# Attention and two MLPs on one core: own buffers for the first batch's queries and keys, the first weight split on three engines, unread products on TensorE

## The chip, the cores and the metric

The kernel runs on one core of a Trainium2 chip. The metric is the device time of one execution in microseconds. The engines are TensorE (PE in the profile, its weight loads PEld), VectorE (DVE), ScalarE (ACT), GpSimd (POOL) and SyncE (SP), which here issues all transfers. Each runs its own list of instructions in order and waits on semaphores.

## The reference

Causal attention with a bias of cumulated sums, over 4 batches of 8 heads, 576 tokens and a head dimension of 64, then two MLPs over the 2304 tokens (512 wide).

```python
scores = scale * np.matmul(q, k.transpose(0, 1, 3, 2))      # q, k, v: (4, 8, 576, 64)
cum = np.cumsum(np.maximum(s, 0.0), axis=-1)
bias = -(cum[:, :, :, None] - cum[:, :, None, :])
scores = np.where(causal, -1000000000.0, scores + np.minimum(bias, 0.0))
x = softmax(scores) @ v                                      # then to (2304, 512)
...
h = x @ w_in                                                 # first MLP, 1024 wide
solu = h * softmax(h)
ln = (solu - mean(solu)) / np.sqrt(var(solu) + 1e-06) * g_ln
x = ln @ w_out
...
h = x @ w2_in                                                # second MLP, 2048 wide
out = (h * np.clip(h + 3.0, 0.0, 6.0) / 6.0) @ w2_out
```

## The kernel before, in words

Products of float32 values are made of three products of rounded parts: each operand is split in a part "hi" (rounded to the type fp32r that TensorE takes) and a part "lo" (the rest), and hi·hi, hi·lo and lo·hi are added up in PSUM. So each weight and each activation has a split: a copy or cast that rounds, and a subtraction.

**Attention in slots.** The work goes by units. A unit is a pair of heads of one batch and one of two kinds: the first kind takes the first 256 queries (two slots), the other the remaining 320 (five slots). There are 32 units, eight for each batch (four of the first kind, then four of the other), and 112 slots. `BASE[u]` is the first slot of unit `u`. Every engine runs a loop over the slot number `n`, and its order in a slot is written out by hand. In slot n TensorE transposes the probabilities of slot n (`transpose_probs`, L687), spreads the reciprocals (`scales`, L724), multiplies with the values (`weighted_values`, L712), does a part of the first MLP, and computes the scores of slot n + 2 (`scores`, L668, L671 for the mask, L673). ACT copies slot n's transposes (L1088) and takes the exponentials of slot n + 1 (L1065). DVE takes the row maximum of slot n + 1 with the bias added (L884) and subtracts for the low part of the probabilities (L893).

**Queries and keys.** They come by `load_qk` on SP, one load for each unit and head of the pair (`load_of(u, e)` = 2u + e), into three buffers in turn, with a wait until the scores of the load three before are done. ACT rounds them (`split_qk`, L1057), POOL subtracts for queries (L555) and keys (L558). `SPLIT_AT` names the slot.

**The bias.** DVE sums s up (L864, L866), SP stores the sums to memory (L473), and loads them back spread over 128 partitions (`load_bias`, L446), behind a wait for the store.

**The first MLP.** It goes in 18 tiles of 128 tokens, from slot 14 on: tile t starts at slot `STARTS[t]` and takes six steps, spread over the slots up to the next start. Steps 0 to 2 are the hidden products (`hidden`, L742: 24 products of 512 columns), steps 3 to 5 the softmax and, from the third tile on, the products with w_out for an earlier tile (`project`, L771). Its input's split is on DVE (L939) and POOL (`split_x`, L604). The weight w_in (512 x 1024) is loaded in four transfers in slots 0, 2, 4, 6. POOL splits it alone, in 16 parts of 256 columns (`split_w_in`: cast L589, subtraction L591), one or two in each slot from slot 3 on; the first hidden product waits for all 16. w_out (L932 on DVE, L1101 on ACT) is split in slots 24 to 31.

**The second MLP** follows behind slot 134 and has TensorE nearly to itself.

Of the kernel before, what the change touches and what calls it, by code (L numbers as in the profile page):

```python
# [14 lines left out]
P = 128  # L15
# [4 lines left out]
F1 = 1024  # L20
# [63 lines left out]
STARTS = [14, 23] + [32 + 7 * i for i in range(4)] + [60 + 6 * i for i in range(8)] + [109, 116, 122, 128, 134]  # L84
# [7 lines left out]
W_IN_PARTS = 16  # L92
W_IN_FROM, W_OUT_FROM, EARLY_FROM = 3, 24, 120

# [40 lines left out]

SUMS_AT = {}
# [34 lines left out]
def build(nc, qk0, qk1, v_rows, s, w_in, w_out, g_ln, w2_in, w2_out, cum_dram, out):  # L171
    with ExitStack() as ctx:
# [35 lines left out]
        qk_hi, qk_raw, qk_lo = [], [], []  # L208
        for p in range(3):
            qk_hi.append(sb(a_region, f"qk_hi{p}", [P, ST], F32R))  # L210
            with nc.sbuf_tensor(f"qk_raw{p}", [P, ST], F32) as raw:
                qk_raw.append(raw)
            qk_lo.append(sb(a_region, f"qk_lo{p}", [P, ST], F32R))
# [16 lines left out]
        w_in_lo = sb(first, "w_in_lo", [P, NC, F1], F32R)  # L230
        w_out_hi = sb(first, "w_out_hi", [P, NF1, DM], F32R)
# [106 lines left out]
        qk_loaded = [sem(f"qk_loaded{p}") for p in range(3)]  # L338
# [4 lines left out]
        w_in_loaded = [sem(f"w_in_loaded{p}") for p in range(NC)]  # L343
# [31 lines left out]
        w_in_split = sem("w_in_split")  # L375
# [43 lines left out]

        def tokens(u):  # L420

            b, p, c = u // (2 * PAIRS), u % PAIRS, kind(u)
            return p, slice(SEQ * b + Q0[c], SEQ * b + Q1[c])

        @block.sync
        def _(sp):
            def load_qk(u, e):
                load = load_of(u, e)
                p, c = load % 3, kind(u)
                if load >= 3:  # L430
# [37 lines left out]

            sp.dma_start(s_pos[:, :], s).then_inc(s_loaded, 16)
# [12 lines left out]
            first_tail = min(u for u in range(UNITS) if not FIRST_KIND[u])  # L482
            load_bias_tail(first_tail)
            for n in range(-2, BASE[UNITS] + 4):

                for load in range(3, 2 * UNITS):
# [47 lines left out]
        def _(pool):  # L534
# [12 lines left out]
            def split_qk(u, e, behind):  # L547

                load, c = load_of(u, e), kind(u)
                p = load % 3  # L550
# [33 lines left out]
            def split_w_in(n):  # L584
                width = NC * F1 // W_IN_PARTS
                raw, hi, lo = (t[:, :, :].rearrange("p c f -> p (c f)")[:, n * width:(n + 1) * width]
                               for t in (w_in_raw, w_in_hi, w_in_lo))
                pool.wait_ge(w_in_loaded[n * NC // W_IN_PARTS], 16)
                pool.tensor_copy(hi, raw).then_inc(w_in_hi_done, 1)  # L589
                pool.wait_ge(w_in_hi_done, n + 1)  # L590
                pool.tensor_tensor(lo, raw, hi.bitcast(F32), ALU.subtract).then_inc(w_in_split, 1)  # L591
                return w_in_split, n + 1
# [24 lines left out]
            w_in_next = 0  # L617
            for n in range(-3, END + 1):
                t, r = STEP_AT.get(n, (None, None))
                if n in SPLIT_X_AT:  # L620
                    behind = split_x(SPLIT_X_AT[n])
# [3 lines left out]
                for u, e in VALUES_AT.get(n, ()):  # L625
                    behind = split_v(u, e)
                if r == 5:
# [17 lines left out]
        def _(pe):  # L645
            def scores(n, part=None):
# [12 lines left out]
                for tile, e, _ in TILES[n]:  # L659
# [3 lines left out]
                    p = load_of(u, part if e is None else e) % 3  # L663
# [148 lines left out]

            pe.wait_ge(consts_done, 4)
            pe.wait_ge(mask_tail_done, 2)
            pe.wait_ge(zeros_done, 1)
            for n in range(-2, END):
# [14 lines left out]
                if 0 <= n + 2 < ITEMS:  # L831
# [5 lines left out]
                    if k == 2:  # L837
                        scores(n + 4, 0)
                if r in (1, 2):
# [22 lines left out]
        def _(dve):  # L862
# [7 lines left out]
            def row_max(n, tile, e, col):  # L870
# [5 lines left out]
                else:  # L876
                    dve.wait_ge(bias_loaded[e][half_of(u)], 16 * len(units_of_half(u)))
# [37 lines left out]
            def scale_pair(u):  # L915
# [12 lines left out]
                last.then_inc(x_done, 1)  # L928

# [52 lines left out]
            for n in range(-2, END + 1):  # L982
# [25 lines left out]
                if n in X_AT:  # L1008
                    split_x(X_AT[n])
# [224 lines left out]
```

## Time and profile before

| | |
|---|---|
| median of 3 runs | 928.36 us (926.16 to 928.52) |
| the profiled execution | 927.4 us, span 925.6 us |
| TensorE busy | 846.5 us (91%), 4912 matmuls |
| DVE, ACT, POOL busy | 437.2, 407.7, 307.9 us |
| granted TensorE clock, mean | 0.972 of 2.4 GHz |

The span is what the profiler saw of the program on the core; the time of the execution has 1.8 us more around it. Busy times are of one execution. A line such as L742 is the line of the kernel that the instruction comes from. The row of a group ends with the idle time of the engine in front of it and what ended it.

### The profile page before, as it was taken

What the parts mean: (1) busy time and instruction counts of PE and PEld (TensorE: products, weight loads), DVE (VectorE), ACT (ScalarE), POOL (GpSimd) and SP (SyncE); (2) the same over time, 40 slices, a digit from 0 to 9 for tenths busy, and PEclk for the clock granted to TensorE, in tenths of its full rate; (3) what the DMA queues carried; (4) which work ended last, traced back from release to release, by engine and by line L of the source; (5) the groups of instructions that cost most, each with busy time, mean ns of one, the idle gap of its engine ahead of it and who ended that gap; (6) DMA issues with size and microseconds to landing.
All of it is one profiled execution on the core that took longest, in us unless ns stands there. A gap on an engine that the chain in (4) does not pass through costs nothing.

```text
span 925.6 us, 13793 instructions
## 1 busy us (share of the span) xinstructions
PE 846.5 (91%) x4912; PEld 753.1 (81%) x4912; DVE 437.2 (47%) x1057; ACT 407.7 (44%) x901; POOL 307.9 (33%) x419
## 2 busy tenths in 40 slices
PE   5676878999899998999898999999999999999997
PEld 4555767878788887788787899999989898989996
DVE  3536677666676767766645232222232322232222
ACT  5636576656755566566323244322232322232222
POOL 5894375545654456545156244000000000000000
PEclk9879879999999999999999999999999999999999
DMA  6736333434333234322212040000000000000000
GB/s 180 222 101 206 99 104 120 136 94 116 119 119 95 85 117 131 108 93 72 72 65 93 1 137 1 35 1 1 34 1 1 35 1 1 35 1 1 35 1 34
DMA packets 39139, 67.11 MB, mean 73 GB/s; under 512 B 4448, under 2 KB 16736, under 8 KB 39072
## 3 DMA queue, kind: packets, MB, share of 16 engines
q1 hardware_dynamic: 39072, 66.23, 23.1%
q8 instruction: 40, 0.66, 0.3%
q14 instruction: 27, 0.22, 0.1%
HBM read 61.42 MB, written 4.79 MB: 72 GB/s over the span
## 4 chain that ended last, share of the span: by engine, by line
PE 71%; DVE 9%; ACT 8%; POOL 6%; issue 5%; DMA 1%; SPq 0%; DVEq 0%; ACTq 0%; POOLq 0%
PE psum L742 10%; PE psum L791 7%; PE psum L793 7%; PE psum L809 7%; PE psum L792 7%; PE psum L810 7%; PE psum L808 7%; PE psum L712 4%; PE psum L687 3%; PE psum L771 3%; DVE es L953 2%; PE psum L673 2%; ACT prob L1065 2%; ACT p_hi L1088 2%; PE psum L668 2%
## 5 line engine op out<-in xcount | busy, mean ns | idle before, releaser
L1019 DVE SCALAR_TENSOR_TENSOR act<-act,psum 128x384 f32<-128x384 f32 x96 | 53.2, 554 | 287.2 <-ACT act L1160 287.2
L1160 ACT ACTIVATE act<-psum,three 128x384 f32<-128x384 f32 x96 | 55.7, 580 | 285.8 <-PE psum L793 285.8
L791 PE MATMUL psum<-x_hi,w_hi 128*128 128x384 f32 x384 | 129.5, 337 | 0.9 <-DVE x_lo L979 0.9
L793 PE MATMUL psum<-x_hi,w_lo 128*128 128x384 f32 x384 | 129.5, 337 | 0.0
L792 PE MATMUL psum<-x_lo,w_hi 128*128 128x384 f32 x384 | 129.0, 336 | 0.0
L810 PE MATMUL psum<-w_hi,g_lo 128*128 128x512 f32 x288 | 113.9, 395 | 0.0
L809 PE MATMUL psum<-w_lo,g_hi 128*128 128x512 f32 x288 | 113.7, 395 | 0.0
L893 DVE TENSOR_TENSOR p_lo<-psum,p_hi 128x512 fp32r<-128x512 f32 (+2 forms) x128 | 71.9, 572 | 86.9 <-ACT p_hi L1088 86.4
L808 PE MATMUL psum<-w_hi,g_hi 128*128 128x512 f32 x288 | 112.0, 389 | 0.0
L1088 ACT ACTIVATE p_hi<-psum 128x512 fp32r<-128x512 f32 (+2 forms) x128 | 62.2, 499 | 111.3 <-PE psum L687 79.8
L771 PE MATMUL psum<-lnT_hi,w_out_hi 128*128 128x256 f32 x288 | 83.3, 289 | 12.4 <-DVE xT L975 12.4
L668 PE MATMUL psum<-qk_hi 128*128 128x128 f32 (+2 forms) x192 | 66.0, 349 | 26.7 <-issue 9.6
L1065 ACT ACTIVATE prob<-prob,nmax 128x128 f32<-128x128 f32 (+4 forms) x144 | 83.2, 579 | 12.6 <-DVE nmax L884 12.4
L555 POOL TENSOR_TENSOR qk_hi<-qk_raw,qk_hi 64x256 fp32r<-64x256 f32 (+1 forms) x64 | 56.6, 885 | 93.6 <-ACT qk_hi L1057 92.4
L687 PE MATMUL psum<-ident,prob 128*128 128x128 f32 x400 | 67.8, 290 | 17.1 <-ACT prob L1065 15.0
L771 PE MATMUL psum<-lnT_lo,w_out_hi 128*128 128x256 f32 x288 | 82.3, 286 | 0.0
L771 PE MATMUL psum<-lnT_hi,w_out_lo 128*128 128x256 f32 x288 | 82.1, 285 | 0.0
L791 PEld LDWEIGHTS psum<-x_hi,w_hi 128*128 128x128 f32 x384 | 72.2, 188 | 5.3 <-DVE x_lo L979 1.1
L792 PEld LDWEIGHTS psum<-x_lo,w_hi 128*128 128x128 f32 x384 | 72.1, 188 | 4.0
L673 PE MATMUL psum<-qk_lo,qk_hi 128*128 128x128 f32 (+2 forms) x192 | 73.9, 390 | 0.0
L884 DVE CUSTOM_DVE_ANT_0 prob<-psum,bias 128x128 f32<-128x128 f32 (+3 forms) x128 | 59.9, 487 | 26.3 <-PE psum L673 20.2
L687 PEld LDWEIGHTS psum<-ident,prob 128*128 128x128 f32 x400 | 50.4, 149 | 26.9 <-ACT prob L1065 21.9
(91 smaller groups left out, 1891.1 us busy)
## 6 DMA issues: line engine op xcount, KB each, us to landing
qk_raw<-qk SPq DMA_DIRECT2D x32, 480.0 KB, 3.5
qk_raw<-qk SPq DMA_DIRECT2D x32, 256.0 KB, 2.7
bias<-cum_dram SPq DMA_DIRECT2D x32, 256.0 KB, 3.9
v_raw<-v_rows SPq DMA_DIRECT2D x32, 160.0 KB, 2.7
bias_tail<-cum_dram SPq DMA_DIRECT2D x32, 144.0 KB, 3.2
out<-out_sb SPq DMA_DIRECT2D x6, 768.0 KB, 3.5
bias<-cum_dram SPq DMA_DIRECT2D x32, 128.0 KB, 3.4
w_raw<-w_in SPq DMA_DIRECT2D x16, 256.0 KB, 3.2
```

The lines of the kernel that those rows point to most:

```text
L668: pe.matmul(ps, q, qk_hi[p][:, keys], start=(part != 1), stop=False)
L673: last = pe.matmul(ps, q, qk_lo[p][:, keys], start=False, stop=(part != 0))
L687: last = pe.transpose(dst, prob[:, src:src + P], ident[:, :])
L742: last = pe.matmul(bank(h_bank(t) + half), x, w, start=(n % 12 == 0), stop=(n % 12 == 11))
L771: last = pe.matmul(bank(L_BANK, PJW), w, x, start=(n == 0), stop=(n == 23))
L791: pe.matmul(ps, w2_hi[f][:, cols], xh, start=(c_ == 0), stop=False)
L792: pe.matmul(ps, w2_hi[f][:, cols], xl, start=False, stop=False)
L793: last = pe.matmul(ps, w2_lo[f][:, cols], xh, start=False, stop=(c_ == NC - 1))
L808: pe.matmul(bank(4 + k), gh, w2_hi[f][:, NC * P:], start=(f == 0), stop=False)
L809: pe.matmul(bank(4 + k), gh, w2_lo[f][:, NC * P:], start=False, stop=False)
L810: last = pe.matmul(bank(4 + k), gl, w2_hi[f][:, NC * P:], start=False, stop=(f == NF2 - 1))
L1065: sc.activation(p, p, ACT.Exp, scale=-1.0, bias=nmax[:, u % 2, col:col + 1], accum_out=rsum[:, u % 2, col:col + 1]).then_inc(exp_done, 1)
```

## The change

Five things change.

- **Own buffers.** The loads 0 to 7 (all of the first kind in the first batch) get a buffer each (`OWN` = 8; `buffer_of`), in a region that the w_out weight takes later. The other loads take the three old buffers in turn. SP's order in front of the loop changes, so that these loads and the first of the wide ones are issued there. SP waits for the scores of the first eight slots before it loads w_out.
- **When queries and keys are split.** ACT's splits for the first batch move ahead (`SPLIT_AT`), others by one slot; POOL does its part one slot behind ACT's, and in front of the values' and the input's split.
- **Unit 0's bias** is not loaded. TensorE spreads it by two products with a column of the identity, into PSUM, and ACT copies it out (`copy_bias`).
- **w_in's split** goes in 8 parts of 512 columns: ACT rounds all (slots 3 to 10), DVE subtracts for the first four (slots 4 to 7), POOL for the last four (slots 8 to 11). It is loaded in 8 transfers, in slots 0 to 7. The hidden products of the first tile wait part by part.
- **Unread products** (`keep_busy`): 24 products of 128 columns at the start of TensorE's list, and 16 behind the scores in each slot from -2 to 11, into a PSUM bank that nobody reads. The first MLP starts at slot 12 instead of 14, and the first products of tile 0 go there (`STARTS`).

```diff
-STARTS = [14, 23] + [32 + 7 * i for i in range(4)] + [60 + 6 * i for i in range(8)] + [109, 116, 122, 128, 134]
+STARTS = [12, 21, 31, 37, 44, 51, 59, 65, 71, 77, 84, 90, 96, 102, 109, 115, 121, 127, 133]
...
-W_IN_PARTS = 16
+W_IN_PARTS = 8
+W_IN_DVE = 4
 W_IN_FROM, W_OUT_FROM, EARLY_FROM = 3, 24, 120
+OWN = HEADS
...
+def buffer_of(load):
+    return 3 + load if load < OWN else (load - OWN) % 3
+def loads_of_buffer(load):
+    return 1 if load < OWN else (load - OWN) // 3 + 1
...
-    SPLIT_AT.setdefault(BASE[_u] - (3 if _u % (2 * PAIRS) <= PAIRS else 4), []).append((_u, 0))
-    SPLIT_AT.setdefault(BASE[_u] - 2, []).append((_u, 1))
+    for _e in range(2):
+        if load_of(_u, _e) < OWN:
+            _n = max(-3, load_of(_u, _e) - 5)
+        elif _u == PAIRS:
+            _n = BASE[_u] - 5 + _e
+        elif _e == 1:
+            _n = BASE[_u] - 3
+        else:
+            _n = BASE[_u] - (4 if _u % (2 * PAIRS) <= PAIRS else 5)
+        SPLIT_AT.setdefault(_n, []).append((_u, _e))
...  SP, ahead of its loop
             load_qk(0, 1)
+            load_qk(1, 0)
             sp.wait_ge(cum_done, 1)
             sp.dma_start(cum_dram, cum[:, :]).then_inc(cum_stored, 16)
-            load_qk(1, 0)
+            load_qk(1, 1)
             sp.wait_ge(cum_stored, 16)
-            for u in range(2):
-                for e in range(2):
-                    load_bias(u, e)
-            for u in range(2):
-                for e in range(2):
-                    load_v(u, e)
+            for e in range(2):
+                load_bias(1, e)
+            load_qk(2, 0)
+            for e in range(2):
+                load_v(0, e)
+            load_qk(2, 1)
+            load_qk(3, 0)
+            for e in range(2):
+                load_v(1, e)
+            load_qk(3, 1)
             first_tail = min(u for u in range(UNITS) if not FIRST_KIND[u])
-            load_bias_tail(first_tail)
+            load_qk(first_tail, 0)
...  SP, in its loop
-                if n in (0, 2, 4, 6):
-                    c_ = n // 2
-                    sp.dma_start(w_in_raw[:, c_, :], w_in[c_ * P:(c_ + 1) * P, :]).then_inc(w_in_loaded[c_], 16)
+                if n in (1, 3):
+                    load_qk(*((first_tail, 1), (first_tail + 1, 0))[n // 2])
+                if n == 2:
+                    load_bias_tail(first_tail)
+                if 0 <= n < W_IN_PARTS:
+                    load_w_in(n)
                 if n == W_OUT_FROM - 6:
+                    sp.wait_ge(scores_ready, OWN)
...  POOL
-            for n in range(-3, END + 1):
+            for n in range(-2, END + 1):
                 t, r = STEP_AT.get(n, (None, None))
-                if n in SPLIT_X_AT:
-                    behind = split_x(SPLIT_X_AT[n])
+                for u, e in SPLIT_AT.get(n - 1, ()):
+                    behind = split_qk(u, e, behind)
...
-                for u, e in SPLIT_AT.get(n, ()):
-                    behind = split_qk(u, e, behind)
-                for _ in range(1 if n < 8 else 2):
-                    if n >= W_IN_FROM and w_in_next < W_IN_PARTS:
-                        behind = split_w_in(w_in_next)
-                        w_in_next += 1
+                i = n - W_IN_FROM - 1
+                if W_IN_DVE <= i < W_IN_PARTS:
+                    behind = split_w_in(i)
...  TensorE
-                    if t == 0:
-                        pe.wait_ge(w_in_split, W_IN_PARTS)
...
+                    if t == 0 and term == 0:
+                        if n // 3 < W_IN_DVE:
+                            pe.wait_ge(w_in_lo_dve, n // 3 + 1)
+                        else:
+                            pe.wait_ge(w_in_lo_pool, n // 3 - W_IN_DVE + 1)
...
+            def keep_busy(n):
+                for _ in range(n):
+                    pe.matmul(bank(H_BANK + 1, P), ident_bf[:, :], mask_bf[:, :], start=True, stop=True)
+
             pe.wait_ge(consts_done, 4)
+            keep_busy(24)
+            pe.wait_ge(cum_done, 1)
+            for e in range(2):
+                pe.matmul(bank(H_BANK + e, CUT), ident[0:NH, e:e + 1].broadcast_to([NH, P]), cum[:, 0:CUT],
+                          start=True, stop=True).then_inc(bias_spread, 1)
...  in its loop, behind the scores
+                if n == -2:
+                    pe.wait_ge(bias_copied, 2)
+                if n < FIRST_STEP:
+                    keep_busy(16)
...  DVE
+            def split_w_in(i):
+                dve.wait_ge(w_in_hi_done, i + 1)
+                dve.tensor_tensor(w_in_part(w_in_lo, i), w_in_part(w_in_raw, i), w_in_part(w_in_hi, i).bitcast(F32),
+                                  ALU.subtract).then_inc(w_in_lo_dve, 1)
...  ACT
+            def copy_bias(e):
+                sc.wait_ge(bias_spread, e + 1)
+                sc.activation(bias[e][:, 0:CUT], bank(H_BANK + e, CUT), ACT.Copy).then_inc(bias_copied, 1)
+
+            def split_w_in(i):
+                sc.wait_ge(w_in_loaded[i], 16)
+                sc.activation(w_in_part(w_in_hi, i), w_in_part(w_in_raw, i), ACT.Copy).then_inc(w_in_hi_done, 1)
...
                 for u, e in SPLIT_AT.get(n, ()):
                     split_qk(u, e)
+                    if (u, e) == (0, 1):
+                        copy_bias(0)
+                        copy_bias(1)
+                if 0 <= n - W_IN_FROM < W_IN_PARTS:
+                    split_w_in(n - W_IN_FROM)
```

## Rows read from the trace of the kernel before

**Rows 1.** The page, its part 1: busy time of each engine.

```profile
PE 846.5 (91%) x4912; PEld 753.1 (81%) x4912; DVE 437.2 (47%) x1057; ACT 407.7 (44%) x901; POOL 307.9 (33%) x419
```

**Rows 2.** Busy time by stretches: length, PE, PEld, DVE, ACT, POOL, clock, DMA share, GB/s.

```profile
0.00:25.00 25.00, 13.84 (x59) 11.53 (x59) 8.22 (x31) 13.05 (x36) 13.25 (x32) 1.00 0.66 183
25.00:65.00 40.00, 25.37 (x137) 20.98 (x135) 20.88 (x62) 22.40 (x54) 37.34 (x61) 0.79 0.53 172
65.00:133.00 68.00, 52.18 (x283) 43.03 (x284) 42.02 (x116) 41.96 (x99) 35.35 (x49) 0.83 0.43 134
133.00:336.00 203.00, 187.53 (x1280) 165.21 (x1280) 140.62 (x363) 123.85 (x285) 109.40 (x151) 0.98 0.37 112
```

**Rows 3.** The chain of waits, of 25 to 65, 65 to 133 and 133 to 336 us.

```profile
by line: POOL w_in_lo L591 24.5%; POOL qk_lo L558 17.6%; POOL w_in_hi L589 13.8%; POOL qk_hi L555 13.8%; issue 10.3%; POOL v_sp L574 9.0%; POOL v_sp L572 4.4%; POOL xs_lo L604 3.1%; POOL wide L580 3.0%; PE psum L742 1.2%; POOLq L552 0.2%; P
...
by line: PE psum L742 16.5%; issue 12.9%; PE psum L712 11.2%; PE psum L687 8.9%; ACT prob L1065 8.3%; ACT p_hi L1088 5.2%; PE psum L668 4.1%; DVE es L953 3.8%; PE psum L673 3.6%; DVE prob L884 2.7%; ACT xT L1096 2.6%; ACT qk_hi L1057 2.3%; 
...
64.98 3.16 PE psum L742 x8
...
162.47 1.85 PE psum L742 x8
```

**Rows 4.** POOL's groups by form, 0 to 70 us: busy us, mean ns.

```profile
L591 POOL TENSOR_TENSOR w_in_lo<-w_in_raw,w_in_hi 128x256 fp32r<-128x256 f32 x16 | 11.7, 733 | 1.3
L558 POOL TENSOR_TENSOR qk_lo<-qk_raw,qk_hi 128x576 fp32r<-128x576 f32 x5 | 7.0, 1404 | 0.4
L589 POOL CAST w_in_hi<-w_in_raw 128x256 fp32r<-128x256 f32 x16 | 6.4, 398 | 0.0
...
L555 POOL TENSOR_TENSOR qk_hi<-qk_raw,qk_hi 64x384 fp32r<-64x384 f32 x5 | 5.0, 1000 | 0.4
...
L604 POOL TENSOR_TENSOR xs_lo<-xT,xs_hi 128x512 fp32r<-128x512 f32 x1 | 1.3, 1298 | 0.0
```

**Rows 5.** TensorE's timeline (start, duration): transposes of slots 0, 8, 31, 32; first hidden product.

```profile
11.29 0.90 PE L687 MATMUL psum<-ident,prob 128*128 128x128 f32 x3 [1.77 <-ACT prob L1065]
...
38.99 0.49 PE L687 MATMUL psum<-ident,prob 128*128 128x128 f32 x3
...
64.98 0.50 PE L742 MATMUL psum<-w_in_hi,xs_hi 128*128 128x512 f32 x1 [2.32 <-POOL w_in_lo L591]
...
128.51 0.90 PE L687 MATMUL psum<-ident,prob 128*128 128x128 f32 x3 [0.95 <-ACT prob L1065]
...
133.13 0.84 PE L687 MATMUL psum<-ident,prob 128*128 128x128 f32 x3
```

**Rows 6.** The timeline of the start, DVE's first row maximum.

```profile
9.92 0.29 DVE L884 CUSTOM_DVE_ANT_0 prob<-psum,bias 128x128 f32<-128x128 f32 x1 [5.18 <-DMA bias<-cum_dram]
```

**Rows 7.** ACT's groups by form, 0 to 70 us: busy us, mean ns.

```profile
L1088 ACT ACTIVATE p_hi<-psum 128x384 fp32r<-128x384 f32 x12 | 5.9, 489 | 16.5 <-PE psum L687 13.5 <-PE psum L712 3.0
...
L1057 ACT ACTIVATE qk_hi<-qk_raw 128x512 fp32r<-128x512 f32 x8 | 5.0, 624 | 2.3 <-DMA qk_raw<-qk 2.3
...
L1065 ACT ACTIVATE prob<-prob,nmax 128x256 f32<-128x256 f32 x8 | 4.0, 496 | 0.0
```

**Rows 8.** The mask product L671: min/median/max ns of its weight load; two timeline rows.

```profile
L671 PEld LDWEIGHTS psum<-mask_bf,ident_bf x128: 95/95/149, 6.6 to 439.3; 128*128 128x128 bf16 x128
...
20.52 0.33 PE L671 MATMUL psum<-mask_bf,ident_bf 128*128 128x128 bf16 x1
20.61 0.56 PE L673 MATMUL psum<-qk_lo,qk_hi 128*128 128x256 f32 x1
```

**Rows 9.** Who waited for whom, 0 to 70 us: us in total, times, longest.

```profile
PE psum L668 <- POOL qk_lo L558: 7.7, 2, 6.4
```

**Rows 10.** DVE's w_out_lo: min/median/max ns; the slowest one's timeline.

```profile
L932 DVE SCALAR_TENSOR_TENSOR w_out_lo<-w_out_raw,g_sb,w_out_hi x8: 712/750/1137, 105.8 to 133.4; 128x512 fp32r<-128x512 f32 x8
...
125.71 0.72 POOL L558 TENSOR_TENSOR qk_lo<-qk_raw,qk_hi 128x256 fp32r<-128x256 f32 x1
...
125.84 1.14 DVE L932 SCALAR_TENSOR_TENSOR w_out_lo<-w_out_raw,g_sb,w_out_hi 128x512 fp32r<-128x512 f32 x1
```

More of the change, by code:

```diff
@@ L208, in build, with qk_buffer @@
         qk_hi, qk_raw, qk_lo = [], [], []
+        def qk_buffer(stack, p, width):
+            qk_hi.append(sb(stack, f"qk_hi{p}", [P, width], F32R))
+            with nc.sbuf_tensor(f"qk_raw{p}", [P, width], F32) as raw:
+                qk_raw.append(raw)
+            qk_lo.append(sb(stack, f"qk_lo{p}", [P, width], F32R))
         for p in range(3):
[L210 to L213, printed above, removed]
+            qk_buffer(a_region, p, ST)
         v_sp = [sb(a_region, f"v_sp{p}", [P, NQ, 2, DH], F32R) for p in range(2)]
@@ L230, in build @@
         w_in_lo = sb(first, "w_in_lo", [P, NC, F1], F32R)
+        with ExitStack() as own:
+            for p in range(3, 3 + OWN):
+                qk_buffer(own, p, QW[1] + KN[1])
         w_out_hi = sb(first, "w_out_hi", [P, NF1, DM], F32R)
@@ L337, in build @@
         cum_stored = sem("cum_stored")
-        qk_loaded = [sem(f"qk_loaded{p}") for p in range(3)]
+        qk_loaded = [sem(f"qk_loaded{p}") for p in range(3 + OWN)]
         v_loaded = [[sem(f"v_loaded{p}{i}") for i in range(2)] for p in range(2)]
@@ L342, in build @@
         bias_tail_loaded = sem("bias_tail_loaded")
-        w_in_loaded = [sem(f"w_in_loaded{p}") for p in range(NC)]
+        w_in_loaded = [sem(f"w_in_loaded{p}") for p in range(W_IN_PARTS)]
         w_out_loaded = sem("w_out_loaded")
@@ L374, in build @@
         w_in_hi_done = sem("w_in_hi_done")
-        w_in_split = sem("w_in_split")
+        w_in_lo_dve = sem("w_in_lo_dve")
+        w_in_lo_pool = sem("w_in_lo_pool")
+        bias_spread = sem("bias_spread")
+        bias_copied = sem("bias_copied")
         w_out_hi_done = sem("w_out_hi_done")
@@ L418, in head_of, with w_in_part, bias_loads @@
             return HEADS * b + 2 * p + e
+        def w_in_part(tensor, i):
+            half, c_ = i // NC, i % NC
+            return tensor[:, c_, half * BANK:(half + 1) * BANK]
+        def bias_loads(u):
+            return len(units_of_half(u)) - (1 if half_of(u) == half_of(0) else 0)
         def tokens(u):
@@ L428, in load_qk @@
                 load = load_of(u, e)
-                p, c = load % 3, kind(u)
-                if load >= 3:
+                p, c = buffer_of(load), kind(u)
+                if load >= OWN + 3:
                     u_, e_ = (load - 3) // 2, (load - 3) % 2
@@ L467, in load_v, with load_w_in @@
                     sp.dma_start(raw[:, :, :], v_rows[h]).then_inc(v_loaded[e][half_of(u)], 16)
+            def load_w_in(i):
+                half, c_ = i // NC, i % NC
+                sp.dma_start(w_in_part(w_in_raw, i),
+                             w_in[c_ * P:(c_ + 1) * P, half * BANK:(half + 1) * BANK]).then_inc(w_in_loaded[i], 16)
             sp.dma_start(s_pos[:, :], s).then_inc(s_loaded, 16)
@@ L471, in _ @@
             load_qk(0, 1)
+            load_qk(1, 0)
             sp.wait_ge(cum_done, 1)
             sp.dma_start(cum_dram, cum[:, :]).then_inc(cum_stored, 16)
-            load_qk(1, 0)
+            load_qk(1, 1)
             sp.wait_ge(cum_stored, 16)
-            for u in range(2):
-                for e in range(2):
-                    load_bias(u, e)
-            for u in range(2):
-                for e in range(2):
-                    load_v(u, e)
+            for e in range(2):
[8 more added lines that the diff above has]
+            load_qk(3, 1)
             first_tail = min(u for u in range(UNITS) if not FIRST_KIND[u])
-            load_bias_tail(first_tail)
+            load_qk(first_tail, 0)
             for n in range(-2, BASE[UNITS] + 4):
-                for load in range(3, 2 * UNITS):
+                for load in range(OWN + 3, 2 * UNITS):
                     u_, e_ = (load - 3) // 2, (load - 3) % 2
@@ L549, in split_qk @@
                 load, c = load_of(u, e), kind(u)
-                p = load % 3
+                p = buffer_of(load)
                 pool.wait_ge(*behind)
@@ L582, in widen @@
                 return wide_done, u + 1
[L584 to L592, printed above, removed]
+            def split_w_in(i):
+                pool.wait_ge(w_in_hi_done, i + 1)
+                pool.tensor_tensor(w_in_part(w_in_lo, i), w_in_part(w_in_raw, i), w_in_part(w_in_hi, i).bitcast(F32),
+                                   ALU.subtract).then_inc(w_in_lo_pool, 1)
+                return w_in_lo_pool, i - W_IN_DVE + 1
             def variance(t):
@@ L662, in scores @@
                     diag0 = tile * P
-                    p = load_of(u, part if e is None else e) % 3
+                    p = buffer_of(load_of(u, part if e is None else e))
                     q = qk_hi[p][:, q_at:q_at + P]
@@ L876, in row_max @@
                 else:
-                    dve.wait_ge(bias_loaded[e][half_of(u)], 16 * len(units_of_half(u)))
+                    if u == 0:
+                        dve.wait_ge(bias_copied, e + 1)
+                    else:
+                        dve.wait_ge(bias_loaded[e][half_of(u)], 16 * bias_loads(u))
                     b_at = u % 2 * CUT if FIRST_KIND[u] else 0
@@ L1054, in split_qk @@
                 load = load_of(u, e)
-                p, w = load % 3, QW[kind(u)] + KN[kind(u)]
-                sc.wait_ge(qk_loaded[p], 16 * (load // 3 + 1))
+                p, w = buffer_of(load), QW[kind(u)] + KN[kind(u)]
+                sc.wait_ge(qk_loaded[p], 16 * loads_of_buffer(load))
                 sc.activation(qk_hi[p][:, 0:w], qk_raw[p][:, 0:w], ACT.Copy).then_inc(qk_hi_done, 1)
```

6 lines of the change are left out of this document (5 added, 1 removed).

## Prediction

> **What bounds the kernel now.** I read the summary of engines, then one table of stretches, then the chain of the stretch from 25 to 65 us with POOL's own groups, and last the timelines of single slots.
>
> TensorE is busy 846.5 of 925.6 us [rows 1]. The table shows where half of the other 79 us lie: it idles 11.2 of the first 25 us, 14.6 of the 40 to 65 us, and 15.8 of the 68 to 133 us, 41.6 together; after that it is busy 187.53 of 203 [rows 2]. In the second and third stretch the granted clock is also 0.79 and 0.83 in the mean, against 0.98 behind them: parts run at 1.2 instead of 2.4 GHz.
>
> From 25 to 65 us the bound is POOL: 37.34 of 40 us busy [rows 2], and the chain there is almost only POOL, the first weight's split (L591, L589) leading with 38% [rows 3]. The split is 16 casts and 16 subtractions, 6.4 + 11.7 = 18.1 us [rows 4]. It ends in front of the first hidden products: TensorE stands 2.32 us until w_in_lo is done and starts them at 64.98 us [rows 5].
>
> From 65 to 133 us no engine leads: the hidden products are 16.5% of the chain, values, transposes and ACT's exponentials take turns behind them [rows 3]. This is a loop through engines, with DVE and ACT 62% busy each [rows 2].
>
> **The change part by part.** I count in slots and take as a slot's start that of its transposes (L687): slot 0 at 11.29, slot 8 at 38.99, slot 32 at 133.13 us [rows 5]. The target is the time of slot 32, since behind it TensorE's work is the same and fills 92% of the time.
>
> *Start, to slot 0.* The first row maximum starts at 9.92 us after DVE has idled 5.18 us for the bias to come back from memory [rows 6], so its scan was done by 4.7. Now two products and two ACT copies spread unit 0's bias. The trace has no such product: at least nothing, at most the 0.4 us of a hidden product of 512 columns at the low clock each (eight in 3.16 us [rows 3]), each doubled as margin for its unrounded operands, so 1.6 us for both; the copies at most 0.5 us each, as a 128x384 copy takes 489 ns [rows 7]. That gives 4.7 + 1.6 + 1.0 = 7.3 instead of 9.9 us. But 24 unread products stand in front of the bias products, and 16 more in each of slots -2 and -1 in front of the first transposes. An unread product is the mask product L671. In the trace the one at 20.52 us is followed by the next product's start after 0.09 us; its weight load alone takes 95 ns at the high clock and 149 at the low [rows 8]. I take 0.07 us each at the high and 0.12 at the low clock, near the start to start, with bounds 0.05 and 0.15. The 24 cost 2.9 us from some 2.4 us on, where TensorE has nothing to do; the 32 cost 2 to 4 us, which eats the gain of 2.6. Slot 0 stays near 11 us: term 0.
>
> *Slots 0 to 7.* Here TensorE waited 7.7 us in two pieces for L558, POOL's part of the keys [rows 9], which came late for want of a free buffer. With own buffers the loads of the whole group go ahead of the loop; unit 2's first is the third of 11 that SP issues once the sums are stored, so it lands before it is asked for. What remains is each engine's own work in a slot. ACT: copy 0.49, exponentials 0.50 and, as the other is half as wide, 0.4, keys 0.62 [rows 7], corrections 0.4, together 2.4 us; from slot 3 on one copy of w_in of 512 columns more, 0.62 (as the keys' of that size), and in slots 3 and 4 wider keys. POOL: keys two subtractions of 256 columns, 0.73 each as L591's of that width, values of 128 columns 0.8 (between half and all of a cast and a subtraction of 256, 0.57 and 1.13), widening 0.2, so 2.5 [rows 4]. TensorE: its 25.37 us from 25 to 65 us at 0.79 of the clock served ten slots, 2.0 each; kinds of narrow tiles are lighter, 1.8; with 16 x 0.07 = 1.1 that is 2.9. This is the longest, against (38.99 - 11.29) / 8 = 3.5 in the trace. Slot 8 starts at 11 + 8 x 2.9 = 34 us instead of 39.
>
> *The weight's split.* POOL sheds 18.1 us and takes back four subtractions of 512 columns at 1.3 us, as xs_lo has this shape [rows 4]: 12.9 us less. ACT gets 8 x 0.62 = 5 us and DVE four subtractions at 0.71 us, w_out_lo's quickest [rows 10], 2.9 us; both are below 60% busy in this stretch [rows 2], and their part of the loop is in the sums above. In slots 8 to 11 POOL still has two loads of keys (2 x (1.00 + 1.40) = 4.8), two of values of 320 columns (2.8, by width from a cast and a subtraction of 256), a widening (0.4), the four subtractions (5.2) and xs_lo (1.3): 14.5 us from 34 on. The hidden products now belong to slot 12 and wait for xs_lo: they start at 48 instead of 65 us. POOL's half of the weight is asked for a slot later.
>
> *Slots 12 to 31.* In the trace 18 slots lie from the first hidden product to slot 32, (133.1 - 65.0) / 18 = 3.8 us each [rows 5]. Now it is 20 slots with the same two tiles, and one step of the third already in slot 31: 48 + 20 x 3.8 = 124. Of this step 1.9 us are work done ahead, and the first eight hidden products, 3.16 us at the low clock, would be 1.3 us shorter at the high one (eight in 1.85 us, both [rows 3]). So 133.1 - 124 + 1.9 + 1.3 = 12.3 us are gained. Unread products end before slot 12. SP's eight transfers of w_in go in slots 0 to 7, half as large as the four before.
>
> *Behind slot 32.* The start slots differ by one or two and meet the old list from the tenth tile on; each tile keeps six steps, and the last 21 slots hold no attention, so that one fewer removes no work. Term 0, with 3 us either way for where the loop and the clock fall.
>
> Sum: 927.4 for the profiled execution (span 925.6 and 1.8 around it) less 12.3 is 915.1; the median of the runs is 1.0 above it, so 916.
>
> **The rivals.**
> *More than this.* The clock stays high through the loop too. By the means in [rows 2] some 40 us between 25 and 133 us are at the low clock (40 x 0.42 + 68 x 0.34). Slots 12 to 31 at 3.4 instead of 3.8 us give 8 more: 908. Against it: the unread products end at slot 12, and the loop's stalls behind it are untouched.
>
> *Given back later.* Hidden products start early, but the slots then run at the pace of the one before slot 32, 4.6 us (128.51 to 133.13 [rows 5]): 48 + 20 x 4.6 = 140, and nothing is left, 925 to 932. For it: the attention in front of the first tile was only moved beside it. Against it: slots 24 to 31 carry the split of w_out, slots 14 to 23 do not.
>
> *Slower: unread products set the slot.* If the clock stays low, 16 take 2.4 us at 0.15 each, and 1.8 us of attention become 3.6: 6 us a slot, 11 + 12 x 6 = 83 us for slot 12, slot 32 at 159 and the end at 951. It decides from a pace of 4.5 us, (65 - 11) / 12. Against it: where TensorE is busy nearly all the time, from 133 us on, the clock is 0.98.
>
> *DVE and POOL hold each other.* w_out_lo took 712 ns at best and 1137 ns once, that time starting 0.13 us behind POOL's L558 [rows 10]. Four DVE subtractions in slots 4 to 7, each held by a POOL instruction of up to 1.4 us [rows 4], are 5.6 us on the loop if nothing hides them: 922. POOL is nearly always busy there, so they will meet; whether TensorE feels it is the doubt. The Trainium skill has this as a rule (SBUF — State Buffer, Who interferes with whom): a VectorE instruction with two inputs in SBUF and a GpSimd one that reads SBUF exclude each other for a whole instruction; the trace agrees, by the one of eight that took 0.43 us longer.
>
> **How the numbers follow.** Forecast 0.50, more 0.20, DVE and POOL 0.13, given back 0.10, slower 0.07. The range 905 to 925 takes in the first three and leaves out "given back", "slower" and the far side of "more", 0.2 in all. A measurement of this kernel can tell 0.3% from no change, 2.8 us. Faster: 0.50 + 0.20 + 0.13 + 0.03 of "given back" = 0.86; same 0.06; slower 0.08.
>
> **What would show it.** Slot 0 near 11 us; slot 8 near 34; the first hidden product near 48, waiting for xs_lo and not for w_in_lo; slot 32 near 124; POOL busy 13 us less; TensorE busy up to 10 us more by 248 unread products, less what the high clock takes off; matmul records of the short kind before 25 us. The prediction fails if slots 0 to 7 take over 3.4 us each, or slots 12 to 31 more than 4.2.

## The result, and the profile after

The changed kernel took 922.19 us in the median of 5 runs (921.63 to 924.8), the kernel before 928.4 us (926.16 to 928.52) beside it; the ratio is 0.9945, interval 0.9925 to 0.9965. So it is faster, by 0.55%, some 5 to 6 us, where 12.3 were forecast; the time itself lies inside the range of 905 to 925. The profiled execution spans 919.8 us, 5.8 less than before. Its trace, like each one here, is of one execution and not of the median; it is the fastest of the five.

The page, part 1, of the changed kernel:

```profile
PE 854.6 (93%) x5164; PEld 762.0 (83%) x5164; DVE 441.8 (48%) x1061; ACT 412.8 (45%) x911; POOL 296.7 (32%) x391
```

POOL sheds 11.2 us and TensorE's busy time grows by 8.1 [rows 1]. The same stretches as in [rows 2]:

```profile
0.00:25.00 25.00, 22.23 (x210) 20.09 (x211) 10.06 (x38) 17.36 (x47) 17.88 (x38) 1.00 0.72 225
25.00:65.00 40.00, 31.70 (x264) 26.25 (x263) 22.75 (x60) 23.42 (x55) 25.23 (x32) 0.91 0.46 140
65.00:133.00 68.00, 51.73 (x291) 42.91 (x290) 48.97 (x130) 44.87 (x107) 36.46 (x53) 0.85 0.49 142
133.00:336.00 203.00, 186.41 (x1292) 164.71 (x1291) 138.86 (x362) 125.97 (x292) 109.40 (x150) 0.99 0.38 112
```

From 25 to 65 us POOL fell from 37.34 to 25.23 us: it is no longer what fills that stretch. What the slots did shows in TensorE's timeline (L736 are the transposes, L794 the hidden products; slots 0, 8, first hidden product, third tile's first hidden product, slot 32):

```profile
13.15 0.50 PE L736 MATMUL psum<-ident,prob 128*128 128x128 f32 x3
...
34.51 0.50 PE L736 MATMUL psum<-ident,prob 128*128 128x128 f32 x3
...
51.94 0.79 PE L794 MATMUL psum<-w_in_hi,xs_hi 128*128 128x512 f32 x1 [3.54 <-POOL xs_lo L655]
...
125.10 0.80 PE L794 MATMUL psum<-w_in_hi,xs_hi 128*128 128x512 f32 x1 [3.78 <-POOL xs_lo L655]
...
129.56 0.49 PE L736 MATMUL psum<-ident,prob 128*128 128x128 f32 x3
```

Slot 8 comes at 34.51 us as forecast (34). But the first hidden product comes at 51.94 instead of 48, after 3.54 us in which TensorE stood for xs_lo, and in slot 31 it stands 3.78 us for the same thing; in the trace before there is no such wait at the third tile. Slot 32 comes at 129.56 where 124 was forecast. Before it was 133.13 [rows 5], so 3.6 us are gained there, and with the 1.9 us of hidden products already done 5.5: that is nearly the whole difference of the spans, 5.8.

Why xs_lo is late is seen in the timeline around slot 12, all engines:

```profile
39.89 1.01 POOL L610 TENSOR_TENSOR qk_hi<-qk_raw,qk_hi 64x384 fp32r<-64x384 f32 x1 [3.17 <-ACT qk_hi L1135]
...
44.90 0.72 DVE L1015 CAST xs_hi<-xT 128x512 fp32r<-128x512 f32 x1
...
46.83 1.28 POOL L641 TENSOR_TENSOR w_in_lo<-w_in_raw,w_in_hi 128x512 fp32r<-128x512 f32 x1
...
48.19 0.99 POOL L610 TENSOR_TENSOR qk_hi<-qk_raw,qk_hi 64x384 fp32r<-64x384 f32 x1
...
49.26 1.40 POOL L613 TENSOR_TENSOR qk_lo<-qk_raw,qk_hi 128x576 fp32r<-128x576 f32 x1
...
50.62 1.26 POOL L655 TENSOR_TENSOR xs_lo<-xT,xs_hi 128x512 fp32r<-128x512 f32 x1
...
56.98 0.69 DVE L955 CUSTOM_DVE_ANT_0 prob<-psum,bias 128x512 f32<-128x512 f32 x1 [7.04 <-PE psum L722]
...
58.85 0.49 ACT L1166 ACTIVATE p_hi<-psum 128x384 fp32r<-128x384 f32 x1 [9.06 <-PE psum L761]
```

Its rounded part is there from 45.6 us. POOL takes a weight part and then the keys of two slots ahead (L610, L613, 2.4 us) in front of it: that is the part of the change that turned POOL's order in a slot around. Before that, from 36.7 us on, POOL stood 3.17 us for the keys that ACT rounds (the row at 39.89); from there on it worked without a pause. TensorE, in order, has the hidden products ahead of the next scores, so DVE's row maxima stood 7.04 us and ACT's copies 9.06 us. And the eight products behind the wait go at the low clock, 0.43 us apart, though 16 unread products had run from 46.1 to 47.2 us.

### The profile page after: what moved, and what is told of

It reads as the page before. It is cut to its first block, busy times and chain, and to the rows that moved or that the text cites. A ratio compares the mean times of both kernels' runs of the same rounds, so it can differ in the third digit from the quotient of the medians.

```text
span 919.8 us, 14285 instructions
## 1 busy us (share of the span) xinstructions
PE 854.6 (93%) x5164; PEld 762.0 (83%) x5164; DVE 441.8 (48%) x1061; ACT 412.8 (45%) x911; POOL 296.7 (32%) x391
## 3 DMA queue, kind: packets, MB, share of 16 engines
q1 hardware_dynamic: 39360, 65.97, 23.3%
## 4 chain that ended last, share of the span: by engine, by line
PE 71%; DVE 10%; ACT 9%; issue 5%; POOL 4%; DMA 1%; DVEq 0%; ACTq 0%; POOLq 0%
PE psum L794 9%; PE psum L843 7%; PE psum L845 7%; PE psum L844 7%; PE psum L861 7%; PE psum L862 7%; PE psum L860 7%; PE psum L761 4%; PE psum L823 4%; PE psum L736 3%; ACT prob L1143 3%; DVE es L1029 2%; ACT p_hi L1166 2%; PE psum L722 2%; PE psum L807 2%
## 5 line engine op out<-in xcount | busy, mean ns | idle before, releaser
L610 POOL TENSOR_TENSOR qk_hi<-qk_raw,qk_hi 64x256 fp32r<-64x256 f32 (+1 forms) x64 | 57.0, 890 | 127.3 <-ACT qk_hi L1135 126.2
L736 PE MATMUL psum<-ident,prob 128*128 128x128 f32 x400 | 64.8, 281 | 15.8 <-ACT prob L1143 12.5
L794 PE MATMUL psum<-w_in_hi,xs_hi 128*128 128x512 f32 x144 | 61.3, 425 | 13.3 <-POOL xs_lo L655 13.3
L613 POOL TENSOR_TENSOR qk_lo<-qk_raw,qk_hi 128x256 fp32r<-128x256 f32 (+1 forms) x64 | 71.0, 1109 | 5.0
L845 PEld LDWEIGHTS psum<-x_hi,w_lo 128*128 128x128 f32 x384 | 72.4, 189 | 0.0
L722 PE MATMUL psum<-qk_lo,qk_hi 128*128 128x128 f32 (+2 forms) x192 | 71.3, 376 | 0.0
```

Of the source, the lines that this page charges most:

```text
L722: last = pe.matmul(ps, q, qk_lo[p][:, keys], start=False, stop=(part != 0))
L736: last = pe.transpose(dst, prob[:, src:src + P], ident[:, :])
L794: last = pe.matmul(bank(h_bank(t) + half), x, w, start=(n % 12 == 0), stop=(n % 12 == 11))
L845: last = pe.matmul(ps, w2_lo[f][:, cols], xh, start=False, stop=(c_ == NC - 1))
```

## The experiments

All medians stand beside the kernel before on the same chip (927.4 to 928.7 us); "ratio" is to it. In the diffs, "..." marks lines left out.

**1. xs_lo first in POOL's slot.**

```diff
+                if n in SPLIT_X_AT:
+                    behind = split_x(SPLIT_X_AT[n])
                 for u, e in SPLIT_AT.get(n - 1, ()):
                     behind = split_qk(u, e, behind)
...
-                if n in SPLIT_X_AT:
-                    behind = split_x(SPLIT_X_AT[n])
```

> POOL takes the input's split (xs_lo) as the first work of its slot, as the kernel before does, instead of behind the keys and the values. Theory A (the gain that is missing was lost because xs_lo comes late: TensorE stood 3.54 us at slot 12 and 3.78 us at slot 31 for it, and the eight hidden products behind each ran at the low clock, 3.4 instead of 1.9 us): xs_lo of tile 0 starts 2.4 us sooner or more (the keys' two subtractions no longer in front of it), the stall at slot 12 falls to about 1 us, that at slot 31 to about 1.5 us; 3 to 6 us faster than the changed kernel, 916 to 919. Theory B (the slots from 12 to 31 run at the loop's own pace, the stalls only fill slack): within 1 us of the changed kernel, 921 to 923.

Measured: 912.78 us, ratio 0.9834 (0.9817 to 0.9852): 9.4 us faster than the changed kernel, more than theory A said. Its timeline, POOL and TensorE, then the third tile and slot 32:

```profile
47.77 1.27 POOL L655 TENSOR_TENSOR xs_lo<-xT,xs_hi 128x512 fp32r<-128x512 f32 x1
...
49.09 0.50 PE L794 MATMUL psum<-w_in_hi,xs_hi 128*128 128x512 f32 x1 [0.98 <-POOL xs_lo L655]
...
118.31 0.79 PE L794 MATMUL psum<-w_in_hi,xs_hi 128*128 128x512 f32 x1 [1.51 <-POOL xs_lo L655]
...
122.42 0.49 PE L736 MATMUL psum<-ident,prob 128*128 128x128 f32 x3
```

The first hidden product comes at 49.09 us and the products are now 0.23 us apart, at the high clock; slot 32 comes at 122.42. These are near the 48 and 124 of the prediction. The two waits are 2.56 and 2.27 us shorter, a third of 3.56 us at 235.46 us is down to 1.18, and the first eight products start 0.23 instead of 0.43 us apart, some 1.5 us in all: 8.7 us together. The two traced executions (914.22 and 921.63 us) differ by less, 7.4 us, of which 7.1 are there by slot 32; the medians differ by 9.4. So these waits are where the time went, but not each microsecond of them reached the end.

**2. The third tile in slot 32 again.**

```diff
-STARTS = [12, 21, 31, 37, 44, 51, 59, 65, 71, 77, 84, 90, 96, 102, 109, 115, 121, 127, 133]
+STARTS = [12, 21] + [32 + 7 * i for i in range(4)] + [60 + 6 * i for i in range(8)] + [109, 116, 122, 128, 134]
```

> The changed kernel with the old start slots from the third tile on (32, 39, ...), the first two at 12 and 21 as changed. Theory A: the third tile's input is whole in slot 30 at the earliest, so a start in slot 31 must wait for it, and a start in slot 32 need not; the 3.78 us stall and most of the 1.5 us of low clock behind it vanish, 8 hidden products (1.9 us) come one slot later: 1 to 4 us faster than the changed kernel, 918 to 921. Theory B: the list of start slots does nothing, 921 to 923.5.

Measured: 917.12 us, ratio 0.9887 (0.9871 to 0.9903), 5 us faster, 0.9 us beyond theory A's far end. The wait at slot 12 stays (3.54 us), those at the third and seventh tile are gone: with a slot more between, xs_lo is there just in time (at the third tile POOL ends it at 124.97 us and the product starts at 125.02).

**3. No unread products.**

```diff
-            keep_busy(24)
...
-                if n < FIRST_STEP:
-                    keep_busy(16)
```

> The changed kernel without any of its 248 unread products. Theory A: in slots 0 to 7 they cost 1.0 us a slot of TensorE at the high clock, but without them matmuls run at the low clock until some time near 25 us, as in the kernel before; POOL and ACT set the pace at 2.4 to 2.5 us, so slot 8 comes at 31 to 34 us instead of 34.5 and slot 0 1 to 3 us sooner; POOL's sum to xs_lo then sets the first hidden product at 49 to 52 us: the same to 2 us faster, 920 to 923. Rival C (the unread products bring the gain by the clock): 3 or more us slower, 925 or more, with slot 8 later than 36 us.

Measured: 920.13 us, ratio 0.9932 (0.9912 to 0.9953), 2 us better in the median, but the interval overlaps that of the changed kernel. Rival C falls. The mask product (L720) in the first 25 us shows what they did, changed kernel and this one (min/median/max ns). Below it stand the changed kernel's bias products (L875), and the slots 0 and 8 of this one:

```profile
L720 PEld LDWEIGHTS psum<-mask_bf,ident_bf x14: 95/98/146, 7.3 to 23.6; 128*128 128x128 bf16 x14
...
5.01 2.07 PE L875 MATMUL psum<-cum,ident 32*128 32x256 f32 x4
```

```profile
L720 PEld LDWEIGHTS psum<-mask_bf,ident_bf x14: 146/146/146, 6.9 to 23.3; 128*128 128x128 bf16 x14
...
9.80 0.90 PE L736 MATMUL psum<-ident,prob 128*128 128x128 f32 x3
...
34.15 0.49 PE L736 MATMUL psum<-ident,prob 128*128 128x128 f32 x3
```

With them the records turn short, the sign of the high clock (the profile's clock column says 1.00 for the first 25 us of all these traces and does not show it). When they do is not fixed. In the changed kernel's trace it is about 13 us; in that of experiment 1, where TensorE has the same list, it is 5.6 us, in the midst of the two bias products (L875):

```profile
5.02 1.36 PE L875 MATMUL psum<-cum,ident 32*128 32x256 f32 x4
...
9.86 0.50 PE L736 MATMUL psum<-ident,prob 128*128 128x128 f32 x3
...
34.97 0.50 PE L736 MATMUL psum<-ident,prob 128*128 128x128 f32 x3
```

So slot 0 comes at 13.15 us in one and at 9.86 in the other, and at 9.80 without unread products. By slot 8 nothing is left of it: 34.51, 34.97 and 34.15 us. Up to there neither the unread products nor the clock that they raise decide anything.

**4. The weight's split on POOL alone.**

```diff
-W_IN_DVE = 4
+W_IN_DVE = 0
...  POOL
             def split_w_in(i):
+                pool.wait_ge(w_in_loaded[i], 16)
+                pool.tensor_copy(w_in_part(w_in_hi, i), w_in_part(w_in_raw, i)).then_inc(w_in_hi_done, 1)
                 pool.wait_ge(w_in_hi_done, i + 1)
...
-                if W_IN_DVE <= i < W_IN_PARTS:
+                if 0 <= i < W_IN_PARTS:
...  ACT
-                if 0 <= n - W_IN_FROM < W_IN_PARTS:
-                    split_w_in(n - W_IN_FROM)
```

> The changed kernel with the first weight's split on POOL alone again (eight casts and eight subtractions of 512 columns, one pair in each of slots 4 to 11), ACT and DVE free of it. By the prediction's sum the split's move was worth 12.9 us of POOL in front of the first hidden product. Theory A: POOL has 8 x 0.7 + 4 x 1.27 = 10.7 us more to do before the first hidden product, of which it idles 5 to 7 us now between 25 and 40 us: the product at 56 to 60 instead of 51.9 us, 4 to 8 us slower, 926 to 930. Rival D (the split's place does not matter, own buffers alone brought the gain): 921 to 924.

Measured: 924.62 us, ratio 0.9961 (0.9942 to 0.998). Slower by 2.4 us in the median, less than theory A's least and a little more than D's, and its interval overlaps that of the changed kernel; the wait at slot 12 is 5.55 us and the first hidden product at 53.76, 1.8 us later and not 4 to 8.

**5. Both mends.** Experiments 1 and 2 in one kernel.

> Both mends together: POOL takes xs_lo first in its slot, and the third tile starts in slot 32. Theory A says that both act on the same stall at the third tile (3.78 us in the changed kernel, still 1.51 us with xs_lo first), and that only xs_lo first acts on the one at slot 12. So most of the later start's 5 us are contained in the other's 9.4: 910 to 914, at most 2.5 us faster than xs_lo first alone (912.8). If the two were independent, it would be 907.5.

Measured: 914.39 us, ratio 0.9856 (0.9835 to 0.9876), not faster than experiment 1 (0.9834), and 7 us from the 907.5 of independent parts. The two act on the same waits. Those of 1.51 us at the third tile and 1.18 us at the seventh, which experiment 1 still has, are gone, and nothing is gained by it: with xs_lo first the earlier start does no harm.

**6. xs_lo first, no unread products.** Experiments 1 and 3 in one kernel.

> xs_lo first, and none of the 248 unread products. Without them the changed kernel got 2 us faster (920.1). If the unread products are a plain cost in slots 0 to 11 (theory C1): again 1 to 3 us faster than xs_lo first alone, 910 to 912. If they hold the clock at its high level up to the first hidden products, which now start after a stall of 0.98 us only (theory C2; those eight took 0.2 us apart, the high clock, in that run): the products at slot 12 fall back to the low clock and it is 0 to 3 us slower, 913 to 916.

Measured: 913.09 us, ratio 0.9846 (0.9823 to 0.987), the same as experiment 1. The rows fit C2 in part: of the eight products at slot 12, behind a wait of 1.23 us, the second and the third start 0.24 us apart, at the high clock, and the rest 0.43 us. In the time neither a cost nor a gain of the unread products is seen.

**7. The first batch's keys in the three shared buffers.**

```diff
 def buffer_of(load):
-    return 3 + load if load < OWN else (load - OWN) % 3
+    return load % 3
 def loads_of_buffer(load):
-    return 1 if load < OWN else (load - OWN) // 3 + 1
+    return load // 3 + 1
...
-                if load >= OWN + 3:
+                if load >= 3:
```

> The changed kernel with the loads of the first batch's queries and keys in the three old buffers again, each with the wait for the scores three loads before, everything else (order of loads, slots of the splits, unread products, w_in's split) as changed. Theory A (own buffers are what lets slots 0 to 7 run at 2.7 us, 3.5 before): the loads 3 to 7 come after scores and 3 us of transfer, slots 0 to 7 take 3.2 to 3.8 us, slot 8 at 37 to 42 instead of 34.5 us, first hidden product at 54 to 58 us, 3 to 7 us slower, 925 to 929. Rival D (the buffers only move slack, POOL's sum sets the first hidden product): the same, 921 to 924.

Measured: 931.23 us, ratio 1.0054 (1.003 to 1.0077): 9 us slower than the changed kernel, and slower than the one before. Theory A has the direction, but all its sizes are passed: 3 to 7 us in the time, slot 8 at 47.18 us where it said 37 to 42. The waits from 0 to 50 us of this kernel:

```profile
POOL qk_hi L610 <- ACT qk_hi L1135: 16.4, 9, 5.7
ACT qk_hi L1135 <- DMA qk_raw<-qk: 12.4, 8, 3.5
```

and of the changed one:

```profile
POOL qk_hi L610 <- ACT qk_hi L1135: 8.0, 5, 3.2
...
ACT qk_hi L1135 <- DMA qk_raw<-qk: 2.4, 3, 1.1
```

ACT waits 12.4 instead of 2.4 us for the loads, and the first hidden product is at 65.11 us (forecast 54 to 58), where the kernel before had it. (The loads' order and the splits' slots are those made for own buffers, so this is the price of the buffers within the changed kernel.)

**8. Unread products in slots 13 to 20 too.**

```diff
                 if n < FIRST_STEP:
                     keep_busy(16)
+                elif FIRST_STEP < n < STARTS[1]:
+                    keep_busy(16, L_BANK)
```

> The changed kernel with 16 unread products more in each of slots 13 to 20 (into another bank of PSUM that is free there), 128 in all, some 8 us of TensorE at the high clock. Between 52 and 85 us TensorE idles some 8 us. If the low clock costs more than the products (the prediction's first rival): 1 to 4 us faster, 918 to 921. If they stand in the loop's way (in order, in front of the next transposes): 2 to 6 us slower, 924 to 928.

Measured: 924.3 us, ratio 0.9957 (0.994 to 0.9975), 2 us above the changed kernel, not clear of it. The clock did rise, from 0.87 to 0.96 in the mean of 52 to 85 us, and no time came of it: no gain is left for the prediction's first rival on this way.

**9. xs_lo first, the split on POOL alone.** Experiments 1 and 4 in one kernel.

> xs_lo first in POOL's slot, and the first weight's split on POOL alone again. In the changed kernel this undoing cost 2.4 us (924.6 against 922.2), with the stall for xs_lo 5.55 instead of 3.54 us. With xs_lo first, the split's cast and subtraction of a slot stand behind xs_lo, but those of the slots before still push it. Theory A: the split's move is worth what it brings xs_lo forward: 1 to 4 us slower than xs_lo first alone (912.8), 914 to 917, stall at slot 12 of 2 to 4 us. Rival D (with xs_lo first the place of the split is free): within 1 us.

Measured: 914.55 us, ratio 0.9851 (0.9824 to 0.9879); 1.8 us above experiment 1, the intervals overlap. Time and wait (3.39 us at slot 12) are in theory A's ranges, but rival D is not excluded, so the split's move is worth some 0 to 3 us.

**10 and 11. xs_lo first, all eight subtractions on DVE (`W_IN_DVE = 8`), or all on POOL (`W_IN_DVE = 0`, ACT's roundings stay).**

> xs_lo first, and all eight subtractions of the first weight's split on DVE (slots 4 to 11), none on POOL. POOL sheds 4 x 1.27 = 5.1 us, of them three in front of xs_lo. Theory A (POOL's sum sets xs_lo, DVE has room): the first hidden product waits no more and starts at 47 to 48 us, 0 to 2 us faster, 911 to 913. Rival E (DVE's subtractions with two operands in SBUF wait for POOL: one of the four took 1.61 us against 0.69 for the others, and delayed a row maximum): slots 8 to 11 get 0.5 to 1 us longer each, first hidden product at 49 to 52 us, 1 to 4 us slower.

> xs_lo first, and all eight subtractions on POOL (slots 4 to 11), none on DVE; ACT's casts stay. POOL has four more of 1.27 us in slots 4 to 7, where it idled some 3 us. Theory A: the first hidden product at 49.5 to 52 us, 0 to 3 us slower than 912.8. Rival E: DVE's row maxima in slots 4 to 7 are no longer late, slot 8 comes at 33 to 34 us and the time is the same or 1 us better.

Measured: 910.12 us, ratio 0.9813 (0.9788 to 0.9838), and 910.77 us, ratio 0.9817 (0.9789 to 0.9845). With all on DVE nothing waits for xs_lo at slot 12, as theory A said; with all on POOL the first hidden product is at 50.26 us after 1.06 us. Rival E falls in the first. In the second its time came true but not its reason: slot 8 is at 38.00 us, later than the 34.97 of experiment 1 and not earlier. The two can't be told from each other nor surely from experiment 1: which of the two engines subtracts shows in no total. The first is the fastest kernel of the study in the median, 18.6 us below the one before beside it.

**12. The kernel before, with xs_lo behind keys and values.** The order of POOL's slot is the one part of the change that it has.

```diff
-                if n in SPLIT_X_AT:
-                    behind = split_x(SPLIT_X_AT[n])
                 for u in range(UNITS):
...
                 for u, e in SPLIT_AT.get(n, ()):
                     behind = split_qk(u, e, behind)
+                if n in SPLIT_X_AT:
+                    behind = split_x(SPLIT_X_AT[n])
```

> The kernel before, with one part of the change alone: POOL takes xs_lo behind the keys and the values of its slot. There the third tile starts in slot 32, one slot behind POOL's part, and tile 0 waits for w_in_lo anyway. Theory A (the order costs only together with the earlier start slots): within 2 us of before, 926 to 930, with no new stall for xs_lo before 240 us over 1.5 us. Rival F (the late xs_lo costs by itself at every tile): 4 or more us slower, 932 and up.

Measured: 936.99 us, ratio 1.0103 (1.0081 to 1.0125), 8.3 us slower. Rival F holds and theory A falls: the late xs_lo costs by itself, with the old start slots too. (In experiment 2 the same slots were late enough; there POOL takes the keys a slot behind ACT's rounding, here it takes them in the same slot and stands 1.11 us for ACT until 136.84 us, in front of the third tile's xs_lo.) Who waited for xs_lo, in this kernel (its trace is of the slowest execution, 940.51 us):

```profile
PE psum L742: 9.1, 5
```

In the kernel before it was one wait of 2.42 us, at 460.79 us, and this one has its like. The four new ones (2.46, 1.76, 0.52 and 1.89 us, at 139.8, 170.5, 199.5 and 256.5 us) are at the third, fourth, fifth and seventh tile, and the stretch from 133 to 336 us has its clock at 0.95 instead of 0.98:

```profile
133.00:336.00 203.00, 181.29 (x1202) 157.88 (x1202) 134.62 (x349) 119.17 (x276) 105.76 (x145) 0.95 0.35 105
```

## Why the prediction was wrong

The direction was right and the size was not: 12.3 us forecast, 5 to 6 measured. Point by point:

*The step that failed* is the end of the weight's split, "14.5 us from 34 on" and "they start at 48", with the "20 x 3.8" of slots 12 to 31 and the "Term 0" of "Behind slot 32". It took POOL's work in slots 8 to 11 as a sum without a pause, and it priced POOL's new order inside a slot at nothing. What the runs showed in its place: of the 14.5 us all but the last weight part, 13.2 us, stand in front of the first hidden product, and with them two pauses, 0.95 us at the start of slot 8 and 3.17 us for the keys that ACT rounds. So it is at 51.94 us and not 48. The new order puts the keys of two slots ahead (2.4 us) in front of xs_lo, at slot 12 and later; that brings a new wait of 3.78 us in slot 31 and one of 3.56 us at the seventh tile, and the eight products behind each of these three waits run at the low clock. Shown from both sides: taking the order out of the changed kernel brings 9.4 us, putting it alone into the kernel before costs 8.3.

Without the order the sum comes out nearly as forecast: 49.09 for 48 us, 122.42 for 124, and 912.8 for 916 in all. For the 48 that is in part luck. Of the sum's 14.5 us, one load of keys (2.4) and one weight part (1.3) come behind xs_lo in experiment 1; and POOL waits there too, 3.16 us for ACT's keys and 0.2 at the start of slot 8, which the sum has not. Two errors of 3 to 4 us cancel there.

*Start, to slot 0*: forecast 11 us, measured 13.15, and 9.86 in the trace of experiment 1 with the same TensorE list. The unread products were priced well (24 in 2.7 us at the low clock, 0.11 each; 16 in 0.95 at the high, 0.06; taken were 0.12 and 0.07). The two bias products took 2.0 us at the low clock (5.01 to 7.01), over the upper bound of 1.6, and 1.36 where the clock rose during them. What slot 0 gains or loses is gone by slot 8.

*Slots 0 to 7*: (34.51 - 13.15) / 8 = 2.7 us where 2.9 was forecast and 3.5 before. The time of slot 8 is right, its reason is not. The 2.9 were TensorE's own work with 1.1 us of unread products. In the trace slots 0 to 2 take 2.0 us each, set by TensorE, and slots 3 to 7 take 2.8 to 3.8, where the chain goes through ACT and DVE; and without unread products slot 8 comes 0.4 us sooner, not the 9 of 8 x 1.1. The 7.7 us of rows 9 were also misread. This row of the kernel before shows the longer piece:

```profile
6.36 0.45 PE L668 MATMUL psum<-qk_hi 128*128 128x128 f32 x1 [6.36 <-POOL qk_lo L558]
```

It is the wait from the program's start to the first scores, in front of slot 0. In slots 0 to 7 TensorE waited 1.38 us for L558 and 3.85 us, in three pieces, for L555. That own buffers matter is shown all the same: without them, in this order of loads, the whole gain is lost (experiment 7).

*The weight's split*: POOL's busy time fell by 11.2 us (forecast 12.9), but the time gained is 0 to 3 us (experiments 4 and 9). With the split gone POOL waited 8.0 us for ACT's keys (the waits in experiment 7); 12.9 us of POOL were not 12.9 us of the path.

*Slots 12 to 31*: forecast 3.8 us a slot, measured (129.56 - 51.94) / 20 = 3.9 with the wait of 3.78 in it, and 3.7 in experiment 1. *8 products at the high clock*: wrong in the changed kernel, where they come behind the wait of 3.54 us; right in experiment 1.

*Rivals.* "More than this" by the clock is not seen (experiment 8). "DVE and POOL hold each other": one of DVE's four subtractions took 1.61 us, the others 0.66 to 0.72. It began 0.20 us behind POOL's:

```profile
35.46 1.27 POOL L641 TENSOR_TENSOR w_in_lo<-w_in_raw,w_in_hi 128x512 fp32r<-128x512 f32 x1 [1.78 <-ACT w_in_hi L1182]
35.66 1.61 DVE L1003 TENSOR_TENSOR w_in_lo<-w_in_raw,w_in_hi 128x512 fp32r<-128x512 f32 x1
...
37.30 0.69 DVE L955 CUSTOM_DVE_ANT_0 prob<-psum,bias 128x512 f32<-128x512 f32 x1
```

With 0.66 us for its own work it began that at 36.6, near the end of POOL's at 36.73; the row maximum stands behind it. The scores of that row maximum are ready at 36.67 us (36.25 + 0.42), so it starts 0.6 us late, and ACT's exponentials and the keys that POOL waits for until 39.89 us come behind it. So the hold is there, and the rule of the Trainium skill quoted with that rival (SBUF — State Buffer, Who interferes with whom) agrees, but it met one of four (two of four in experiment 1, 1.90 and 1.62 us), not all, and can't be told in the total (experiments 10 and 11). That this rival's 922 us is just what was measured is luck: it priced four holds at 5.6 us and knew nothing of the order. "Given back later" took part of the gain, by another way than its text, at single waits and not in the pace. "Slower" did not come: the clock rose by 13 us, and slots 0 to 7 took 2.7 us each.

What stays open: experiments 1 and 7 and the rest do not add up to the total (of two parts experiment 5 shows that they act on the same waits), and no run separates the earlier splits of the keys on ACT from the own buffers that allow them, undoes the bias by products alone, or moves the first tile back from slot 12.

## What to carry to other kernels

When a change reorders an in-order engine's list, price each moved instruction by who waits for it next, not only the engine's sum: a 1.3 us subtraction moved behind work that was not urgent (at slot 12, 2.4 us of it) cost 8 to 9 us. What a whole pipeline waits for should be first in its slot. Starting the stage a slot later helped while the subtraction was late (5 us) and brought nothing once it was first. Work taken off a busy engine is worth what it was in front of: some 11 us of POOL's busy time here brought 0 to 3 us. And a sum of one engine's work is a forecast only where the engine does not wait; look for the waits before adding up.

## What the runs showed of the hardware

Unread products bring TensorE to the high clock early: matmul records of 229 instead of 330 ns from 5.6 us on in one execution and from about 13 us in another with the same TensorE list, where without them all are long up to 23.3 us. Behind waits of 3.54 and 3.78 us the products ran at the low clock, behind one of 0.98 us at the high; behind one of 1.23 us, without unread products before it, they fell to the low clock at the third. The total showed no gain from it. A product of two float32 operands that are not rounded shows as two records of 629 to 791 ns each: two products of 256 columns took 2.0 us at the low clock. A DVE subtraction of two SBUF operands started during POOL's took 1.61 us for 0.66.
